# Second expert layer: token turns one product sooner, and the third block addition ahead of two multiplications

## What is computed

```python
def _moe_ref(x, w_gate, w1, w2):
    ...
    for e in range(E):
        h = np.maximum(x @ w1[e], 0.0)
        ye = h @ w2[e]
        out += P[:, e:e + 1] * ye
    return out.astype(np.float32)

def _moe2_ref(x, w_a, w_b, w_out):
    a = x @ w_a
    b = x @ w_b
    return (a * b @ w_out).astype(np.float32)
```

## Time and profile before

| | |
|---|---|
| median of 3 runs | 1452.02 us (1451.71 to 1453.65) |
| the profiled execution | 1450.18 us, its span 1448.4 us |
| TensorE matmul busy | 1398.6 us, 97% of the span |
| TensorE weight loads busy | 1246.1 us, 86% |
| VectorE busy | 808.4 us, 56% |
| ScalarE busy | 501.5 us, 35% |
| GpSimd busy | 223.7 us, 15% |
| chain that ended last | TensorE 86%, VectorE 7%, ScalarE 4%, issue 2% |

### The profile page before, as it was taken

How to read it: one execution, slowest core, us unless ns; L and a number is a source line. 1 busy time by engine, 2 the same in 40 slices (tenths; PEclk the granted TensorE clock), 3 DMA queues, 4 the chain that set the end, 5 groups by cost and what they waited for, 6 DMA issues and landing times.

```text
span 1448.4 us, 20715 instructions
## 1 busy us (share of the span) xinstructions
PE 1398.6 (97%) x7400; PEld 1246.1 (86%) x7400; DVE 808.4 (56%) x1585; ACT 501.5 (35%) x1085; POOL 223.7 (15%) x289
## 2 busy tenths in 40 slices
PE   4877999999999999999999999999999999999999
PEld 3655889988889998889998888998888989999998
DVE  6898765645444453544545444454544666656665
ACT  5785232423223242222323222242322443232331
POOL 3355110101101010110101011010111321101100
PEclk9999999999999999999999999999999999999999
DMA  4311100001010000101001010000100001001002
GB/s 141 100 45 56 44 30 29 30 29 59 15 44 29 29 29 29 58 21 37 29 29 32 26 58 29 29 29 29 58 15 29 15 30 44 30 30 44 30 1 88
DMA packets 49724, 56.45 MB, mean 39 GB/s; under 512 B 2432, under 2 KB 37376, under 8 KB 49664
## 3 DMA queue, kind: packets, MB, share of 16 engines
q1 hardware_dynamic: 44768, 53.26, 11.3%
q10 hardware_dynamic: 4896, 2.41, 0.6%
HBM read 52.51 MB, written 3.15 MB: 38 GB/s over the span
## 4 chain that ended last, share of the span: by engine, by line
PE 86%; DVE 7%; ACT 4%; issue 2%; DMA 0%; DVEq 0%; ACTq 0%
PE ps L623 28%; PE ps L625 28%; PE ps L624 28%; ACT pr L967 2%; DVE pr L1298 1%; DVE st L1675 1%; DVE pr L1272 1%; DVE wsl L1336 1%; PE ps L693 1%; DVE pt L1307 1%; ACT pt L976 1%; PE ps L567 0%; ACT st L1139 0%; ACT hh L1146 0%; DVE acc L1714 0%
## 5 line engine op out<-in xcount | busy, mean ns | idle before, releaser
L623 PE MATMUL ps<-xoh,wsh 128*128 128x384 f32 x1232 | 414.9, 337 | 3.0 <-DVE xol L1579 2.1
L625 PE MATMUL ps<-xol,wsh 128*128 128x384 f32 x1232 | 412.7, 335 | 0.0
L624 PE MATMUL ps<-xoh,wsl 128*128 128x384 f32 x1232 | 412.3, 335 | 0.0
L623 PE MATMUL ps<-w2h,hh 128*128 128x512 f32 x912 | 360.7, 396 | 0.8 <-DVE acc L1557 0.8
L625 PE MATMUL ps<-w2l,hh 128*128 128x512 f32 x912 | 359.8, 395 | 0.0
L624 PE MATMUL ps<-w2h,hl 128*128 128x512 f32 x912 | 359.6, 394 | 0.0
L1562 DVE SCALAR_TENSOR_TENSOR acc<-ps,g_now,acc 128x512 f32<-128x512 f32 x180 | 135.1, 751 | 201.7 <-PE ps L625 201.7
L623 PEld LDWEIGHTS ps<-xoh,wsh 128*128 128x128 f32 x1232 | 231.3, 188 | 10.5 <-DVE st L1675 3.9
L624 PEld LDWEIGHTS ps<-xoh,wsl 128*128 128x128 f32 x1232 | 231.3, 188 | 3.7
L625 PEld LDWEIGHTS ps<-xol,wsh 128*128 128x128 f32 x1232 | 231.2, 188 | 0.0
L625 PEld LDWEIGHTS ps<-w2l,hh 128*128 128x128 f32 x912 | 171.7, 188 | 39.8
(11 more groups left out here) (142 smaller groups left out, 1337.8 us busy)
## 6 DMA issues: line engine op xcount, KB each, us to landing
raw<-in_w_dram SPq DMA_DIRECT2D x32, 512.0 KB, 3.4
raw<-in_w_dram SPq DMA_DIRECT2D x16, 1024.0 KB, 5.1
rk<-in_k_dram SPq DMA_DIRECT2D x8, 384.0 KB, 4.0
rq<-in_q_dram SPq DMA_DIRECT2D x8, 384.0 KB, 4.9
raw<-in_w_a_dram SPq DMA_DIRECT2D x6, 512.0 KB, 3.6
raw<-in_w_b_dram SPq DMA_DIRECT2D x6, 512.0 KB, 3.6
raw<-in_w_out_dram SPq DMA_DIRECT2D x6, 512.0 KB, 3.5
out_dram<-acc SPq DMA_DIRECT2D x12, 256.0 KB, 2.0
```

What stands on the lines that cost most here:

```text
L623: nc.tensor.matmul(o, ah, bh, start=first, stop=False, skip_group_check=True)
L624: nc.tensor.matmul(o, al, bh, start=False, stop=False, skip_group_check=True)
L625: return nc.tensor.matmul(o, ah, bl, start=False, stop=last, skip_group_check=True)
```

## The change

On TensorE, turns 16 and 23 no longer stand behind a product of their own, and the turns between them move up by one product: turn 16 follows turn 15 behind P6, turn 17 stands behind P3, 18 behind P7, 19 behind P1 of sub 1, 20 behind P5, 21 behind P2, and 22 and 23 together behind P6. P3 and P7 of sub 1 have no turn behind them. ScalarE's casts and VectorE's lowerings of the turns move in their programs to match. In every step of the second layer, VectorE does addition 3 of sub 1 right behind addition 2, ahead of multiplications 2 and 3; before, the order was addition 2, multiplication 2, addition 3, multiplication 3.

```diff
-            for x, name in enumerate(FULL):
+            LEAD_TURNS = {"P1": (12,), "P5": (13,), "P2": (14,), "P6": (15, 16), "P3": (17,), "P7": (18,)}
+            FIRST_TURNS = {"P1": (19,), "P5": (20,), "P2": (21,), "P6": (22, 23)}
+            for name in FULL:
                 gated_product(name, 0, 0)
-                turn_sums(12 + x)
+                for v in LEAD_TURNS[name]:
+                    turn_sums(v)
             for k in range(KT):
-                for x, name in enumerate(FULL):
+                for name in FULL:
                     gated_product(name, 1, k)
                     if k == 0:
-                        turn_sums(18 + x)
-                    if k == 0 and x == 0:
+                        for v in FIRST_TURNS.get(name, ()):
+                            turn_sums(v)
+                    if k == 0 and name == "P1":
                         gated_product("P4", 0, 0)
...
             keep_a("P6", 0, 1)
-            for v in (15, 16, 17):
+            for v in (15, 16, 17, 18):
                 x2_hi(v)
             for k in range(KT):
                 first = k == 0
                 keep_b("P1", k, 0)
                 if first:
-                    x2_hi(18)
+                    x2_hi(19)
                     keep_a("P4", 0, 3)
                 keep_b("P5", k, 2)
                 if first:
-                    x2_hi(19)
                     x2_hi(20)
+                    x2_hi(21)
                 keep_b("P6", k, 1)
-                if first:
-                    x2_hi(21)
-                    wo_hi(0)
-                gated_hi(k, 0)
                 if first:
                     x2_hi(22)
                     x2_hi(23)
+                    wo_hi(0)
+                gated_hi(k, 0)
                 gated_hi(k, 1)
...
             add_a(0, 0)
-            x2_lo(14)
-            x2_lo(15)
+            for v in (14, 15, 16):
+                x2_lo(v)
             add_a(0, 1)
-            x2_lo(16)
+            x2_lo(17)
             add_a(0, 2)
-            for v in (17, 18, 19, 20):
+            for v in (18, 19, 20):
                 x2_lo(v)
             for k in range(KT):
                 t = k // B
                 add_b(k, 0)
+                if k == 0:
+                    x2_lo(21)
                 gated(k, 0)
                 if k > 0:
                     gated_lo(k, 0)
                 if k == 0:
-                    x2_lo(21)
                     x2_lo(22)
+                    x2_lo(23)
                 add_b(k, 1)
+                add_b(k, 2)
                 gated(k, 1)
-                if k == 0:
-                    x2_lo(23)
-                add_b(k, 2)
                 gated(k, 2)
```

## The result

| | before | changed |
|---|---|---|
| median | 1451.71 us (1450.80 to 1453.65, 5 runs) | 1444.9 us (1443.57 to 1445.55, 5 runs) |
| profiled execution | 1450.18 us, span 1448.4 | 1443.57 us, span 1441.8 |

The ratio is 0.9954, with a 95% interval of 0.9944 to 0.9965: 5.1 to 8.1 us faster. The forecast was made from a before of 1452.02, the one beside this measurement is 1451.71; as a gain, the range was 3.1 to 7.0 us.

A forecast was written before the change was run, and what follows sets the result against it. TensorE, busy 97% of the span, was taken as the bound, so gains come from its stops. Third addition 3.4 plus turns 2.3 make 5.7 us: profiled 1444.5, plus 1.84 to the median, forecast 1446.3 us, range 1445.0 to 1448.9.

The forecast's parts named there:

- The stop at the second batch's P1: TensorE waits there on a lowering of turned tokens, costing 2.35 us; issuing turns one product sooner was to gain 2.3.
- the two small terms that were set against each other: At the turns on TensorE: turn 16 waits some 0.15 us, two restarts behind turns save 0.17; taken to cancel.
- The short stops: Steps 1 to 10: P4's weight load waits for VectorE's third addition; moving that addition ahead was to gain 3.4 us.
- That is 0.32 us lost: Step 1, P1's last matmul to P4's second: 0.67 us against 0.35 undisturbed; applied to nine steps, with 0.53 for step 5.
- 0.07 to spare, thin: Step 1: moved third addition frees P4's weight load at 1203.21, its turn being 1203.28.
- The row of the expert layer: Same product sequence there, addition right behind P7, loads without a gap; taken as evidence that the whole 3.4 us goes.
- The cover of the pushed-back multiplication: Multiplications come 0.5 us later; 1.7 us between the step's last lowering and the output product hides this, cost nothing.
- The total: Both parts of the change together, 3.4 + 2.3 = 5.7 us gained, forecast 1446.3 us.
- VectorE's queue by rows, not by the page's rule: Independent VectorE operations start 0.48 us apart by rows, 0.55 by the rule; nine steps come out alike either way.
- the 0.1 that the prediction named: Under the page's rule for VectorE's queue, step 5 would keep about 0.1 of its 0.53 us loss.
- The slower rival: Third addition let go at P1's end: 0.7 us more lost in each of ten steps, 1456.7 us; chance 0.03.
- the second one: Rival: short stops shrink but stay, TensorE restarting late at about 0.15 us a step, 1447.8 us; chance 0.10.

The follow-up runs named there:

- fill of 128x128: Changed kernel with an unused 128x128 fill on VectorE between the wait for P7 and the third addition, steps 1 to 11: 1445.39 us.
- P4 a product sooner: Changed kernel with P4 of sub 1 directly behind P7 and the next step's P1 behind it, steps 0 to 10: 1455.88 us.
- the two maxima: Changed kernel with an unused maximum over 192 or 384 columns on VectorE before the third addition, steps 1 to 11: 1446.65 and 1448.72 us.
- turn 23 behind P3: Changed kernel with turn 23 one product later on TensorE, leaving one product (P7) ahead of the second batch's P1: 1445.31 us.
- maximum over 384 columns: Changed kernel with an unused maximum over 384 columns on VectorE between the wait for P7 and the third addition, steps 1 to 11: 1448.72 us.

## Why the prediction was right

**The direction and both mechanisms** were right, and the parts add up as forecast. Point by point:

- *The stop at the second batch's P1*: 2.3 forecast, 2.30 measured. That the sum fits this closely is partly luck. Of the two small terms that were set against each other, turn 16 waited 0.13, not 0.15, and the two restarts (0.17) did go; but the sum took a turn as 0.36 in a pair as well, and a pair takes 0.79, 0.07 more than two turns of 0.36. Two pairs eat 0.14 of the 0.17. So read, the terms give 2.35 + 0.17 - 0.13 - 0.14 = 2.25, and 0.05 is assigned to nothing. Lowering 23 ended at 1176.01 and P1 started at 1176.42: the slack is 0.41, where 0.35 was counted.
- *The short stops*: 3.4 forecast, 3.63 measured. The step of the sum that was sized too small is "That is 0.32 us lost", taken between P1's last matmul and P4's second. It misses that P4 stays uneven behind a late start, at 0.17 to 0.19 a matmul in the kernel before, and that rows with two decimals were subtracted. (3.63 - 0.53) / 9 is 0.34 a step.
- *0.07 to spare, thin*: 0.06, and it held in all ten steps. The row of the expert layer, where an addition stands directly behind P7, foretold it. The fill of 128x128 shows how thin: 0.02 late after 0.08 more.
- *The cover of the pushed-back multiplication*: 1.7 us forecast, 1.72 measured and unchanged. Multiplication 2 starts 0.47 behind the third addition, as counted.
- *The total*: 5.7 forecast, 5.93 in the layer, 6.8 and 6.4 in medians. The range's low end, 1445.0, was set with half a microsecond for the medians; the stages ahead of the layer vary by more (2.1 us among the profiles), so this term of the range was too small.
- *VectorE's queue by rows, not by the page's rule*: pairs of multiplications run 0.46 apart at a duration of 0.55 (1.01 for two, above), and the maximum of 0.35 is followed at 0.27. In nine steps the time decides nothing, since the addition waits for P7 either way. Step 5 decides: there the first multiplication is late, and the queue is what the additions wait for. In the changed kernel they follow the lowering of block 1 at 0.48 and each other at 0.48 (1.03 for two of 0.55), and P4 is not late:

```profile
1290.46 0.56 DVE L1697 TENSOR_TENSOR hl<-st,hh 128x384 fp32r<-128x384 f32 x1 [0.58 <-ACT hh L1150]
1290.94 1.03 DVE L1677 TENSOR_TENSOR st<-ps,st 128x384 f32<-128x384 f32 x2
```

  With each start 0.55 or 0.56 behind the last, the third addition would have ended at 1292.12 and P4's load come at 1292.17, 0.09 behind its turn at 1292.08, the 0.1 that the prediction named. The measured starts speak against the rule of the Trainium skill ("VectorE: DVE Perf Modes", "The DRAIN you can't avoid") that the next operation waits for the pipe to be empty. But the same paragraph goes on that a next operation that is not held starts earlier. The prediction left this sentence out, and these rows agree with it.

The slower rival, an addition let go one product late, is not what happened: the addition starts with P7's end. But its price was of the right kind. With P4 a product sooner, the same distance is missing, and the kernel is slower than before, by 4.9 us. Both rivals that price a late load have it too high: the slower one adds 0.1 for the restart to the 0.94 of lateness, and the second one puts 0.15 on a load that comes 0.03 late. Measured, 0.99 late cost 0.94 and 0.02 late cost 0.01.

## What to carry to other kernels

A busy share of 97% does not say that nothing is left: list the waits of the bounding engine, and for each one the queue of the engine that ends it. An operation that the bounding engine needs next goes ahead of one that only a later stage needs, but it can start only when its own input is there, so count the gain up to that point. And for a hand-over through two more engines, count the chain (here 0.6 + 0.6 + 0.7 us, and 0.2 for the hand-overs between them) against the work that stands between it and its user: one product of 1.1 us was too few, two were enough.

## What the runs showed of the hardware

A weight load that waits for a block addition goes 0.05 us after the addition's end (steps 1 to 10 of the fill and of the two maxima, 0 to 10 with P4 sooner). This is not so for every wait: behind lowering 23 it took 0.12 (1177.77 to 1177.89 with turn 23 behind P3). The loss at a late P4 is its load's lateness behind its turn less 0.04 to 0.05, at 0.20, 0.40 and 0.99 us alike. I had put a single estimate on the restart and expected 0.06.

The cause of one oddity stays open. In step 5 of the kernel before, the first multiplication sits idle for 0.47 us behind the addition whose result it reads, and it does in the changed kernel as well:

```profile
1289.32 0.56 DVE L1685 TENSOR_TENSOR st<-st,ab 128x384 f32<-128x384 f32 x1 [0.47 <-DVE st L1677]
```

Before, it made the stop of step 5 longer (0.53 instead of 0.34); now it is hidden. No run was made for it, but the traces at hand say where it hangs. All nine traces in which VectorE has as many instructions as before have it at step 5. The three with one instruction more in each of steps 1 to 11 do not: they have it at step 8, here with the maximum over 384 columns.

```profile
1360.92 0.56 DVE L1687 TENSOR_TENSOR st<-st,ab 128x384 f32<-128x384 f32 x1 [0.46 <-DVE st L1679]
```

So it moves with the number of instructions ahead of it in VectorE's program, and not with the step or its data. Why that place costs half a microsecond, no run shows.
